# Seven products of half size for the first product of the last stage, in blocks of 640 tokens, with split weight sums kept in DRAM

## The chip, the core and the metric

The kernel runs on one NeuronCore of a Trainium2 chip. The metric is the device time of one execution in microseconds (us). Before the change three runs gave 993.5, 996.51 and 996.72 us; their median is 996.51 us.

The engines: TensorE (PE in the profile; PEld is its weight load), VectorE (DVE), ScalarE (ACT), GpSimd (POOL) and SyncE (SP), which here only issues transfers.

## The reference

Three stages follow one another; each takes the output of the one before.

```python
# 1: attention with a decay, B=4, H=8, S=576, D=64
scores = scale * q @ k.T
out = (scores * gamma ** rel, where rel >= 0) @ v            # -> x (2304, 512)
# 2: mixture of experts, E=8, F=1024, two experts for each token
logits = x @ w_gate;  noise_scale = log1p(exp(x @ w_noise))
top2 of logits + noise_scale * noise;  w = softmax(top2)
out[token] += w * (relu(x @ w1[e]) @ w2[e])                   # -> x (2304, 512)
# 3: the last stage, F2=2048
h = x @ w_in                                                  # (2304, 2048)
return (h * cos(h)) @ w_out                                   # (2304, 512)
```

All is fp32. The kernel keeps the accuracy by splitting: each operand of a large product is written as a high part, rounded to TensorE's fp32r format, and a low part, the rest. A product then takes three matrix products: high x high, low x high, high x low.

## The kernel before, in words

**Order.** Each engine has one program, written out by hand; semaphores order them. An engine does its instructions in the order of its program, so an instruction that waits holds up all behind it. SP issues its transfers in program order too, all on one queue.

**Attention** (to about 130 us) also fills the tables that route the tokens. It scatters the rows of x to slots in DRAM, sorted by expert (`x_slots`).

**Experts** (about 130 to 575 us). The work is cut into units: one expert and 640 slots. A unit goes through the eight 128-wide parts `f` of the hidden width. For each `f` TensorE does `product1` (L1303, 24 matmuls of 320 columns) of the next part and `product2` (L1321, 15 matmuls of 512 columns) of this one, and for `f` under 5 it transposes one tile of 128 rows for the next unit (L1209). ScalarE does `relu`, then `w_high` (L674), which rounds the next expert's weight chunk, 128x1024, and `x_high` (L634). VectorE does the low parts: `h_low` (L1032), `w_low` (L1038) and `x_low` (L1017). SP loads the chunks (`load_ring`, L435) and the rows (`load_rows`, L429), and stores a unit's results to `y_slots` (`store_rows`, L442). The results go out at the end of a unit, and the 256 KB loads `gath` for the unit after next's transposes come behind these stores in SP's order.

**The last stage** (from 576 us). Blocks of 384 tokens (`TPB` = 3 tiles of 128). GpSimd gathers the two result rows of each token (L586); ScalarE and VectorE weigh and add them (`prepare` L731, `combine` L1109). TensorE transposes the sum (L1394), and `prepare_high` (L737) and `combine_low` (L1116) split it. Then for each of the 16 parts `f` of the hidden width `mlp_step` does:

- TensorE: 12 matmuls of 384 columns into one of four PSUM banks (L1458), then 9 of 512 columns (L1477) of the part three steps back (`MLP_LAG`).
- ScalarE and VectorE, for one part of `h`: round `h/2pi` to whole turns (L797, L1165), subtract them (L1168), `Abs` (L802), `Sin` with a bias of pi/2 (L804), the product with h (L1173), and the split of the result (L809, L1176). These steps depend on each other in this order.
- The 16 weight chunks of this stage are loaded and split into `w_hi`, `w_lo`, `w2_hi` and `w2_lo` (`w_high_last` L755, `w_low_last` L1054) during the last unit and the first block. They stay in SBUF for all six blocks.

## Time and profile before

| what | us |
|---|---|
| three runs | 993.5, 996.51, 996.72 |
| profiled execution | 993.64 |
| its span | 991.7 |
| busy TensorE | 973.3 (98%) |
| busy VectorE | 486.5 (49%) |
| busy ScalarE | 425.3 (43%) |
| last stage, first product to the last matmul's end | 575.99 to 987.0 |

1.94 us of the execution lie around the span. "Busy" of TensorE counts from a matmul's start to its modelled end. The matmuls overlap, so the mean duration of one is longer than the distance from one start to the next; what a matmul costs in a row of them is read from the chain of waits, as the length of a piece divided by its count.

### The profile page before, as it was taken

What the parts mean: (1) busy time and instruction counts of PE and PEld (TensorE: products, weight loads), DVE (VectorE), ACT (ScalarE), POOL (GpSimd) and SP (SyncE); (2) the same over time, 40 slices, a digit from 0 to 9 for tenths busy, and PEclk for the clock granted to TensorE, in tenths of its full rate; (3) what the DMA queues carried; (4) which work ended last, traced back from release to release, by engine and by line L of the source; (5) the groups of instructions that cost most, each with busy time, mean ns of one, the idle gap of its engine ahead of it and who ended that gap; (6) DMA issues with size and microseconds to landing.
All of it is one profiled execution on the core that took longest, in us unless ns stands there. A gap on an engine that the chain in (4) does not pass through costs nothing.

```text
span 991.7 us, 17311 instructions
## 1 busy us (share of the span) xinstructions
PE 973.3 (98%) x6108; PEld 879.6 (89%) x6108; DVE 486.5 (49%) x944; ACT 425.3 (43%) x779; POOL 104.1 (10%) x106
## 2 busy tenths in 40 slices
PE   8999899999999999999999989999999999999997
PEld 7989789898989988898989979999999999999996
DVE  4788644333334333433434475555555555555554
ACT  1445334233233332332334465555455554545553
POOL 2276500000000000000000231000000001010000
PEclk9999999999999999999999999999999999999999
DMA  9988444436263542626315641010010101010000
GB/s 363 345 321 302 162 165 154 160 109 212 82 225 114 159 168 97 221 95 196 125 71 175 225 164 43 22 46 30 21 53 21 53 21 42 32 42 21 32 0 33
DMA packets 64359, 122.02 MB, mean 123 GB/s; under 512 B 5696, under 2 KB 31552, under 8 KB 64320
## 3 DMA queue, kind: packets, MB, share of 16 engines
q1 hardware_dynamic: 58080, 101.05, 29.7%
q0 software_dynamic: 6240, 20.45, 6.2%
q8 instruction: 25, 0.41, 0.2%
q14 instruction: 14, 0.11, 0.0%
HBM read 83.73 MB, written 37.75 MB: 122 GB/s over the span
## 4 chain that ended last, share of the span: by engine, by line
PE 86%; DMA 5%; issue 3%; POOL 2%; SPq 2%; DVE 1%; ACT 1%; ACTq 0%; POOLq 0%; DVEq 0%
PE ps L1458 20%; PE ps L1477 20%; PE ps L1303 15%; PE ps L1321 14%; PE ps L1209 2%; DMA gath<-x_slots 2%; PE ps L1339 2%; PE ps L1224 2%; PE ps L1407 2%; PE ps L1351 2%; PE ps L1247 2%; PE ps L1419 2%; DMA y_slots<-y_sb 1%; PE ps L1239 1%; POOL x_slots L540 1%
## 5 line engine op out<-in xcount | busy, mean ns | idle before, releaser
L1303 PE MATMUL ps<-xs,w_hi 128*128 (+1 forms) x784 | 182.9, 312 | 0.0
L1038 DVE TENSOR_TENSOR w_lo<-raw,w_hi 128x1024 fp32r<-128x1024 f32 x48 | 58.8, 1225 | 170.8 <-ACT w_hi L674 170.8
L1303 PEld LDWEIGHTS ps<-xs,w_hi 128*128 128x128 f32 x784 | 133.1, 188 | 0.8
L1458 PE MATMUL ps<-x_hi,w_hi 128*128 (+1 forms) x384 | 130.8, 341 | 0.1
L1458 PE MATMUL ps<-x_hi,w_lo 128*128 (+1 forms) x384 | 129.1, 336 | 0.0
L1458 PE MATMUL ps<-x_lo,w_hi 128*128 (+1 forms) x384 | 129.1, 336 | 0.0
L797 ACT ACTIVATE turns<-ps 128x384 f32<-128x384 f32 x96 | 47.2, 491 | 184.2 <-PE ps L1458 184.2
L1303 PE MATMUL ps<-xs,w_lo 128*128 (+1 forms) x392 | 121.2, 309 | 0.0
L1165 DVE TENSOR_SCALAR turns<-turns 128x384 f32<-128x384 f32 x96 | 37.3, 388 | 168.1 <-ACT turns L797 168.1
L1477 PE MATMUL ps<-w_hi,g_hi 128*128 128x512 f32 x288 | 112.6, 391 | 2.1 <-DVE g_lo L1176 2.1
L1477 PE MATMUL ps<-w_hi,g_lo 128*128 128x512 f32 x288 | 113.3, 393 | 0.0
L1477 PE MATMUL ps<-w_lo,g_hi 128*128 128x512 f32 x288 | 113.3, 393 | 0.0
L674 ACT ACTIVATE w_hi<-raw 128x1024 fp32r<-128x1024 f32 x48 | 50.8, 1059 | 141.3 <-PE ps L1321 107.8
L1321 PE MATMUL ps<-w_hi,hs_lo 128*128 128x512 f32 x245 | 96.2, 393 | 0.0
L1321 PE MATMUL ps<-w_lo,hs_hi 128*128 128x512 f32 x245 | 96.2, 393 | 0.0
L1321 PE MATMUL ps<-w_hi,hs_hi 128*128 128x512 f32 x245 | 95.8, 391 | 0.0
L668 ACT ACTIVATE hs_hi<-ps 128x320 fp32r<-128x320 f32 x98 | 42.3, 437 | 79.3 <-PE ps L1303 79.3
L1458 PEld LDWEIGHTS ps<-x_hi,w_hi 128*128 128x128 f32 x384 | 72.1, 188 | 3.7 <-issue 0.5
L1458 PEld LDWEIGHTS ps<-x_hi,w_lo 128*128 128x128 f32 x384 | 72.1, 188 | 3.1
L1303 PEld LDWEIGHTS ps<-xs,w_lo 128*128 128x128 f32 x392 | 73.7, 188 | 0.8
L1458 PEld LDWEIGHTS ps<-x_lo,w_hi 128*128 128x128 f32 x384 | 72.1, 188 | 0.0
L586 POOL DMA_INDIRECT y<-y_slots,pos_now x42 | 41.8, 995 | 276.3 <-PE ps L1394 266.9
(167 smaller groups left out, 1649.4 us busy)
## 6 DMA issues: line engine op xcount, KB each, us to landing
raw<-weights SPq DMA_DIRECT2D x80, 512.0 KB
y_slots<-zeros_sb SPq DMA_DIRECT2D x42, 256.0 KB, 3.6
gath<-x_slots SPq DMA_DIRECT2D x40, 256.0 KB, 3.5
y_slots<-y_sb SPq DMA_DIRECT2D x40, 256.0 KB, 2.1
qk<-qk SPq DMA_DIRECT2D x18, 512.0 KB
kv<-kv SPq DMA_DIRECT2D x18, 512.0 KB
out<-out_sb SPq DMA_DIRECT2D x18, 256.0 KB, 2.1
x_slots<-zeros_sb SPq DMA_DIRECT2D x8, 256.0 KB, 7.7
```

The source lines that it names most:

```text
L586: nc.gpsimd.indirect_dma_start(out=y[j][:, :], out_offset=None, in_=y_slots, in_offset=bass.IndirectOffsetOnAxis(ap=pos_now[:, k, j:j + 1] ...
L668: nc.scalar.activation(hs_hi[:, par, half * HALF:(half + 1) * HALF], ps[5 + half][:, 0:HALF], ACT.Relu).then_inc(relu_done, 1)
L674: nc.scalar.activation(w_hi[:, f * CHUNK:(f + 1) * CHUNK], raw[:, f % 2, :], ACT.Copy).then_inc(hi_done, 1)
L797: nc.scalar.activation(turns[f % 2][:, :], h_bank(f)[:, 0:TB], ACT.Copy, scale=PER_TURN, bias=ROUND).then_inc(turn_done, 1)
L1038: tt(w_lo[:, at], raw[:, f % 2, :], w_hi[:, at].bitcast(F32), ALU.subtract).then_inc(split_done, 1)
L1165: ts(whole[:, :], whole[:, :], -ROUND, None, ALU.add).then_inc(whole_done, 1)
L1209: last_one = nc.tensor.transpose(x_bank(g, j)[:, k * BLK:(k + 1) * BLK], gath[j][:, k * P:(k + 1) * P], ident)
L1224: last_one = nc.tensor.matmul(ps[half][0:C, n * C:(n + 1) * C], qk_sb[t % 3][rows, 1, n, :], qk_sb[t % 3][rows, 0, n, :], start=True, stop ...
L1303: last_one = nc.tensor.matmul(ps[5 + half][:, 0:HALF], w[:, at:at + P], xs[:, bass.ds(g % 2, 1), a, k, half * HALF:(half + 1) * HALF].rear ...
L1321: last_one = nc.tensor.matmul(ps[j][:, :], a[:, f % 2, j * BLK:(j + 1) * BLK], w[:, at:at + DM], start=f == 0 and i == 0, stop=f == FE - 1 ...
L1458: last_one = nc.tensor.matmul(h_bank(f)[:, 0:TB], w[:, cols], a[:, bass.ds(par, 1), k, :].rearrange("p a s -> p (a s)"), start=k == 0 and ...
L1477: last_one = nc.tensor.matmul(ps[j][:, :], a[f2 % 2][:, rows], w[:, cols], start=f2 == 0 and i == 0, stop=f2 == FT - 1 and i == 2)
```

## The change

**Arithmetic.** The first product of the last stage is written as a product of 2 x 2 blocks: x is cut by tokens and by the 512 features into halves, `w_in` by features and by pairs of 128-wide hidden parts. A scheme of Strassen's kind (with sums that are shared, in Winograd's way) then needs seven products of blocks, where the plain one needs eight, and sums of the operands and of the results. `h` comes out as h1, h2, h3 and h4, the four quarters for two parts and two halves of the tokens.

**Blocks.** `SIZES = (3, 5, 5, 5)`: a first block of 384 tokens, done with plain products, then three of 640 with the scheme, so halves of 320 columns. A *slot* is one pair of hidden parts of one block; there are 8 to a block and 32 in all. `p` is the number of the slot in its block.

**Weights.** The 2 x 2 blocks of each pair, their four sums and all low parts are made during units 1 to 4 of the experts stage (`pair_high`, `pair_low`), from a buffer `raw_pair`, and written to DRAM (`w1_pairs`, `w2_pairs`) by SP (`next_pair`). The last stage reads them again for every slot (`load_w1`, `load_w2`). The splits of the last unit and the first block are gone. The factor 1/2pi is folded into the gates, 2pi into the copy of the results, and the subtraction of whole turns is one instruction of VectorE, where it was two. The gather copies no indices ahead of it. The loops over blocks are written out.

```diff
+SIZES = (3, 5, 5, 5)
...
+A11, A12, A22, S3, S2, S4, S1 = range(0, 7 * Q_W, Q_W)
...
+ORDER = ((A11, 0), (A12, 1), (S2, 4), (S3, 5), (A22, 6), (S1, 3), (S4, 2))
...
+DRAINED = (0, 1, 2, 3, 4, 6, 7)
...
+            def store_pair(i):
+                sp.wait_ge(pair_lo, 3 * (i + 1))
+                sp.dma_start(w1_pairs[i], stage1[i % 2][:, :, :].bitcast(F32)).then_inc(pair_out[i % 2], 16)
+                sp.dma_start(w2_pairs[i], stage2[i % 2][:, :, :].bitcast(F32)).then_inc(pair_out[i % 2], 16)
...
+            def next_pair(i):
+                store_pair(i)
+                if i + 2 < FP:
+                    load_pair(i + 2)
...
                     load_ring(g, f, e_next)
+                    if isinstance(g, int) and 1 < g <= PREP_UNITS + 1 and f == 1:
+                        next_pair(2 * (g - 1) - 1)
+                    if isinstance(g, int) and g <= PREP_UNITS and f == 5:
+                        next_pair(2 * (g - 1))
...
+            def load_w1(slot):
+                if slot >= 2:
+                    sp.wait_ge(p_done, products_before(slot - 1))
+                cols = slice(0, A_W) if slot < FP else slice(Q_W, 2 * A_W)
+                sp.dma_start(w1_of(slot).bitcast(F32), w1_pairs[slot % FP][:, :, cols]).then_inc(w1_in[slot % 2], 16)
```

TensorE's seven products of a slot:

```diff
+            def strassen(slot, o):
+                b, i, n = slot // FP, products_before(slot) + o, HALVES[slot // FP]
+                at, m = ORDER[o]
+                if o == 0:
+                    pe.wait_ge(w1_in[slot % 2], 16 * (slot // 2 + 1))
+                if slot % FP == 0:
+                    pe.wait_ge(x_lo_done, 7 * (b - 1) + o + 1)
+                if slot == FP and o < 2:
+                    pe.wait_ge(g_done, i - 1)
+                elif o == 2:
+                    pe.wait_ge(p1_copied, slot - FP + 1)
+                else:
+                    back = (i - 2 - products_before(FP)) // 7
+                    pe.wait_ge(drained, 7 * back + DRAINED[(o - 2) % 7])
+                w, x = w1_of(slot), x_of(b)
+                for k in range(2):
+                    cols = slice(at + k * P, at + (k + 1) * P)
+                    for j, (hl, a) in enumerate(((0, 0), (1, 0), (0, 1))):
+                        last_one = nc.tensor.matmul(p_bank(i)[:, 0:n], w[:, hl, cols], x[:, a, m, k, :],
+                                                    start=k == 0 and j == 0, stop=k == 1 and j == 2)
+                last_one.then_inc(p_done, 1)
...
+            BEHIND = {10: (1, 1, 2, 1, 2, 2, 1), 6: (1, 1, 1, 1, 1, 1, 0)}
```

VectorE's order in a slot of 640 tokens (`p_done` comes from TensorE, `turn_done` and `sin_done` from ScalarE):

```diff
+                    reduce(slot - 1, 3)
+                    g_low(slot - 1, 2)
+                    product(slot - 1, 3)
+                if slot < SLOTS:
+                    dve.wait_ge(p1_copied, slot - FP + 1)
+                    drain(slot, 1, h_sb[0], p1_sb)
+                if slot > FP:
+                    g_low(slot - 1, 3)
+                if slot == SLOTS:
+                    for j in range(1, SIZES[NBK - 1], 2):
+                        rows_out(NBK - 1, j)
+                    break
+                if p == 1 and b > 1:
+                    rows_out(b - 1, 3)
+                reduce(slot, 0)
+                drain(slot, 2, u2, p1_sb)
+                product(slot, 0)
+                g_low(slot, 0)
+                dve.wait_ge(drained, drained_before(slot) + 2)
+                drain(slot, 3, u3, u2)
+                if p == 0 and b > 1:
+                    rows_out(b - 1, 1)
+                if b + 1 < NBK:
+                    ahead(b, p)
+                dve.wait_ge(drained, drained_before(slot) + 3)
+                drain(slot, 4, h_sb[1], u3, True)
+                reduce(slot, 1)
+                drain(slot, 5, u4, u2)
+                drain(slot, 5, h_sb[2], u3)
+                product(slot, 1)
+                reduce(slot, 2)
+                g_low(slot, 1)
+                dve.wait_ge(drained, drained_before(slot) + 5)
+                drain(slot, 6, h_sb[3], u4)
+                if p == 0 and b == 1:
+                    rows_out(0, 1)
+                product(slot, 2)
```

`ahead(b, p)` makes the split tokens of the next block; VectorE's share of it in block 0 from slot 5 on, and then in blocks 1 and 2:

```diff
+                    if p == 5:
+                        x2_low(1, 0)
+                    if p == 6:
+                        x2_low(1, 1)
+                        for i in range(4):
+                            x2_sum(1, i)
+                    if p == 7:
+                        for at in range(2, 7):
+                            x2_low(1, at)
```

```diff
+                    if p < 5:
+                        combine(first + p)
+                    if p == 4:
+                        x2_low(b + 1, 0)
+                        x2_low(b + 1, 1)
+                    if p == 5:
+                        x2_sum(b + 1, 0)
+                        x2_sum(b + 1, 1)
+                    if p == 6:
+                        x2_sum(b + 1, 2)
+                        x2_sum(b + 1, 3)
+                        x2_low(b + 1, 2)
+                    if p == 7:
+                        for at in range(3, 7):
+                            x2_low(b + 1, at)
```

In block 0 VectorE's order for a slot is `product` and `g_low` of the last slot's second part, `reduce`, `product` and `g_low` of part 0, `ahead`, `reduce` of part 1; ScalarE follows the same order with `turn`, `cosine` (Abs and Sin) and `g_high`. `second` is the old L1477 for one tile and one hidden part: 3 matmuls of 512 columns. `BEHIND` says how many of them follow each of the seven products; there are 10 in a slot of 640 tokens and 6 in one of 384. `drain` is an addition of VectorE that takes a product out of its PSUM bank (two banks, `ps5` and `ps6`, in turn); the first product is copied by ScalarE (`p1_copied`).

The first place is TensorE in the last stage: the end of one step of `mlp_step` before. `x_hi` and `x_lo` are the split tokens, `w_hi` and `w_lo` the weights, `g_hi` and `g_lo` the split h cos(h).

```order
L1458 MATMUL ps<-x_hi,w_hi 128x384
L1458 MATMUL ps<-x_hi,w_lo 128x384
L1458 MATMUL ps<-x_lo,w_hi 128x384
L1466 REGISTER_ALU
L1477 MATMUL ps<-w_hi,g_hi 128x512 [waits g_split]
L1477 MATMUL ps<-w_lo,g_hi 128x512
L1477 MATMUL ps<-w_hi,g_lo 128x512
```

And the same engine within a slot of the block of 640 tokens, with the changed order:

```order
L1831 MATMUL ps<-x_odd,w_sb 128x320 x6
L1749 MATMUL ps<-table_sb,y_2 128x128 x4
L1831 MATMUL ps<-x_odd,w_sb 128x320 x6
L1845 MATMUL ps<-w_sb,g_hi 128x512 x2
L1845 MATMUL ps<-w_sb,g_lo 128x512
L1831 MATMUL ps<-x_odd,w_sb 128x320 x6
```

What stood as 12 and 9 matmuls in a row now stands as 6 and 3, or 6 and twice 3; a transpose (L1749) falls between two products.

The second place is VectorE in the loop over blocks before: one step, with the split of a transposed tile.

```order
L1165 TENSOR_SCALAR turns<-turns 128x384 [waits turn_done]
L1168 SCALAR_TENSOR_TENSOR angle<-ps,turns 128x384 [waits g_split,whole_done]
L1173 TENSOR_TENSOR angle<-ps,angle 128x384 [waits sin_done]
L1176 TENSOR_TENSOR g_lo<-angle,g_hi 128x384 [waits g_hi_done]
L1116 ISA [waits x2_hi_done]
L1116 TENSOR_TENSOR x_lo<-ps,x_hi 128x4x128
```

Its counterpart is the middle of the last slot of block 1, where the split tokens of block 2 (`x_even`) are made:

```order
L1440 TENSOR_TENSOR angle<-h_sb,angle 128x320 [waits sin_done]
L1445 TENSOR_TENSOR g_lo<-angle,g_hi 128x320 [waits g_hi_done]
L1425 TENSOR_TENSOR u<-ps,u 128x320 [waits p_done,drained]
L1380 TENSOR_TENSOR x_even<-xT_sums,x_even 128x640 [waits x_hi_done] x3
L1380 TENSOR_TENSOR x_even<-xT_raw,x_even 128x640 [waits x_hi_done]
L1423 TENSOR_TENSOR h_sb<-u,ps 128x320 [waits p_done,drained]
L1434 SCALAR_TENSOR_TENSOR angle<-turns,h_sb 128x320 [waits g_split,turn_done]
L1425 TENSOR_TENSOR u<-ps,u 128x320 [waits p_done]
```

The drains (L1425, L1423) that set TensorE's banks free now stand in one queue with the four instructions of 640 columns, and behind waits for ScalarE (`sin_done`, `g_hi_done`).

The third place is SP at the start of a unit of the experts stage, with the change:

```order
L522 DMA gath<-x_slots 128x512
L528 ISA [waits split_done]
L528 DMA raw<-weights 128x1024
L569 DMA w_pairs<-stage_1 128x4096 [waits pair_lo]
L570 DMA w_pairs<-stage_1 128x2048
L565 DMA raw_pair<-pairs 128x2048 [waits pair_lo]
L522 ISA [waits tx_done]
L522 DMA gath<-x_slots 128x512
```

Before, the two `gath` stood there with only a `raw` between them; now two stores and a load of a weight pair go ahead of the third `gath`.

## Rows read from the trace of the kernel before

**Rows 1.** The page: busy engines, GB/s in 40 slices of the span, chain by engine.

```profile
PE 973.3 (98%) x6108; PEld 879.6 (89%) x6108; DVE 486.5 (49%) x944; ACT 425.3 (43%) x779; POOL 104.1 (10%) x106
...
GB/s 363 345 321 302 162 165 154 160 109 212 82 225 114 159 168 97 221 95 196 125 71 175 225 164 43 22 46 30 21 53 21 53 21 42 32 42 21 32 0 33
...
PE 86%; DMA 5%; issue 3%; POOL 2%; SPq 2%; DVE 1%; ACT 1%; ACTq 0%; POOLq 0%; DVEq 0%
```

**Rows 2.** Windows: us, busy PE, PEld, DVE, ACT, POOL, granted clock, DMA share, GB/s.

```profile
0.00:100.00 100.00, 96.64 (x1361) 87.38 (x1361) 73.37 (x194) 42.58 (x71) 45.90 (x44) 1.00 0.91 331
565.00:575.00 10.00, 8.92 (x56) 7.52 (x55) 5.68 (x9) 4.55 (x10) 1.85 (x2) 1.00 0.59 201
776.00:848.00 72.00, 72.00 (x370) 65.39 (x369) 37.92 (x75) 37.19 (x76) 5.88 (x7) 1.00 0.11 33
```

**Rows 3.** Chain of waits, experts stage: start, length, what.

```profile
232.60 2.74 DMA gath<-x_slots
...
250.48 0.44 PE ps L1209 x4
250.91 3.52 PE ps L1303 x24
254.44 3.44 PE ps L1321 x15
```

**Rows 4.** Chain of waits, start of the last stage and its steady part.

```profile
552.75 1.41 PE ps L1419 x6
...
575.99 4.43 PE ps L1458 x24
...
586.05 2.33 PE ps L1477 x9
...
603.37 2.07 PE ps L1477 x9
605.44 2.09 PE ps L1458 x12
...
613.78 0.44 PE ps L1394 x4
```

**Rows 5.** Groups by form, experts stage: count, busy us, mean ns, idle before.

```profile
L1038 DVE TENSOR_TENSOR w_lo<-raw,w_hi 128x1024 fp32r<-128x1024 f32 x41 | 50.2, 1225 | 144.1 <-ACT w_hi L674 144.1
L1032 DVE SCALAR_TENSOR_TENSOR hs_lo<-ps,hs_hi 128x320 fp32r<-128x320 f32 x81 | 38.5, 485 | 36.2 <-ACT hs_hi L668 36.2
L1017 DVE TENSOR_TENSOR xs<-ps,xs 128x512 f32 x25 | 17.0, 682 | 0.0
...
L668 ACT ACTIVATE hs_hi<-ps 128x320 fp32r<-128x320 f32 x80 | 34.6, 437 | 64.4 <-PE ps L1303 64.4
```

**Rows 6.** Groups by form, last stage.

```profile
L804 ACT ACTIVATE angle<-angle,table_sb 128x384 f32<-128x384 f32 x96 | 59.2, 617 | 3.1
L1173 DVE TENSOR_TENSOR angle<-ps,angle 128x384 f32<-128x384 f32 x96 | 53.4, 557 | 7.8 <-ACT angle L804 0.5
L802 ACT ACTIVATE angle<-angle 128x384 f32<-128x384 f32 x96 | 49.6, 516 | 0.0
L1109 DVE SCALAR_TENSOR_TENSOR y<-y,gate 128x512 f32<-128x512 f32 x21 | 15.8, 751 | 4.2 <-ACT y L731 2.4
```

**Rows 7.** Timeline of VectorE, last stage, instructions that wait for nothing.

```profile
592.56 0.55 DVE L1173 TENSOR_TENSOR angle<-ps,angle 128x384 f32<-128x384 f32 x1
593.02 0.55 DVE L1176 TENSOR_TENSOR g_lo<-angle,g_hi 128x384 fp32r<-128x384 f32 x1
```

**Rows 8.** Chain of waits at the end: hand-overs ScalarE to VectorE to TensorE.

```profile
979.46 0.02 issue
979.48 0.47 DVE angle L1173
...
980.52 0.04 issue
```

**Rows 9.** Timeline of the end: the copies of the results.

```profile
987.03 1.08 ACT L793 ACTIVATE out_sb<-ps 128x512 f32<-128x512 f32 x2 [3.50 <-PE ps L1477]
```

792 lines of the change are left out of this document (521 added, 271 removed).

## The prediction, made before the changed kernel ran

> **What bounds the kernel now.** I read the page first. TensorE is busy 98% and is 86% of the chain that ended last; VectorE is half idle [rows 1]. By windows the last stage has TensorE busy for all of 72 us, VectorE for 37.9, ScalarE for 37.2, at 33 GB/s and at a granted clock of 1.00, the 2.4 GHz level [rows 2]. So TensorE's work sets the time there, and work taken from it counts as long as the others keep up. What a matmul costs in a row I take from the chain: 24 of 320 columns in 3.52 us (0.147 each), 15 of 512 in 3.44 (0.230) [rows 3], 12 of 384 in 2.09 (0.174), 9 of 512 in 2.07 (0.230) [rows 4].
>
> **Products, -19.4 us.** For 640 tokens and a pair of hidden parts the plain first product costs 24 x 0.174 x 640/384 = 6.97 us. The new one has 7 x 6 = 42 matmuls of 320 columns, 6.16 us. That is 0.81 less in each of 24 slots, 19.4 in all: an eighth less work, of which the narrower matmuls give back a bit. The second product (30 x 0.230 = 6.90 a slot), the first block and the 18 transposes stay. A slot of 640 tokens is then 13.06 us of TensorE, 13.5 with a transpose (0.44) [rows 4].
>
> **More seams.** Groups are now of 6 and 3 matmuls. A group of 9 costs 2.07 and one of 15 costs 3.44, the same 0.230 each, so a seam costs nothing there; one of 6 took 1.41, up to 0.03 over 6 x 0.230 [rows 3, 4]. With some 10 seams more a slot the bounds are 0 and 24 x 10 x 0.03 = 7 us. I take 0, by the larger groups.
>
> **Do VectorE and ScalarE keep up?** This decides the case. The trace shows no drain, so I price it by VectorE's 0.485 at 320 columns. A copy on ScalarE is 0.437 at 320; Abs and Sin fall from 0.516 and 0.617 at 384 to about 0.46 and 0.56, by the slope of copies [rows 5, 6]. A hand-over between engines takes 0.02 to 0.04 [rows 8]; I take 0.04. Independent instructions of VectorE start 0.46 apart while one lasts 0.55 [rows 7], so at 320 I take 0.42.
>
> In a slot VectorE has 7 drains, 4 `reduce`, 4 `product`, 4 `g_low`: 19 x 0.42 = 8.0 us of 13.06. But its order makes one long chain with ScalarE. From `product` 3 of one slot: drain 1, turn, reduce, Abs, Sin, product 0, g_high, g_low, drains 3 and 4, turn, reduce, Abs, Sin, product 1, g_high, g_low, drain 6, turn, reduce, Abs, Sin, and `product` 3 again. The durations sum to 10.9, 20 hand-overs to 0.8: 11.7 us, 1.3 under TensorE's 13.06. So bare slots (all of block 3) run at TensorE's pace.
>
> The work for the next block stands in that chain, ahead of drain 4. An instruction of 640 columns lies between 0.682 (512) and 1.225 (1024) [rows 5]; by the slope 0.82, or 0.76 from start to start. The chain grows to:
>
> - p=0 to 3: 12.4 to 13.6 against 13.5; about even.
> - p=4: a combine (0.751 [rows 6]) and two lows behind ScalarE: 14.1 against 13.5, 0.6 over.
> - p=5: two sums, 13.2 against 13.1, 0.1 over.
> - p=6: two sums and a low, 14.0, 0.9 over.
> - p=7: four lows, 14.7, 1.7 over.
>
> That is 3.3 over. TensorE takes a bank two products after it was filled; the tightest of these waits, for `p1_copied`, has 0.9 us in hand. So TensorE stands about 2.5 us before each of blocks 2 and 3: **+5 us**. In block 0 a slot is 8.35 us (24 x 0.174 + 18 x 0.230) and the chain 6.7, with 1.9 over in p=6 (a low and four sums, 4.0 us) and 1.6 in p=7 (five lows, 3.9). And the last `reduce` of the block stands behind those five lows. The second product of slot 8 waits for its `product` (g_done): by my times that comes 4.3 us late. **+4.3 us**. The bounds of these 9.3 us: 0, if waits that I add up overlap; 30, if hand-overs cost more (a rival below).
>
> **Start of the last stage, -1.9 us.** Before, TensorE stood 1.1 us of the 10 before the stage [rows 2], waiting for gathered rows. The gather starts about 0.9 us sooner without its index copy, and no weight chunks share the DMA engines with it: -1.1. Then four products of 2.09 would end at 584.35, but the first second product starts at 586.05 [rows 4]: 1.7 lost while weights are split on ScalarE and VectorE. Now none are split there, but with two banks the third product must wait for the whole chain of the first, about 0.9. -0.8. Bounds of both: -2.8 and 0.
>
> **End, -0.5 us.** Two copies took 1.08 us after the last matmul [rows 9]; now the other tiles end sooner and one copy is left, about 0.6. The chain of the last quarter needs 4.1 us and has 5.5 of second products ahead.
>
> **Weight pairs in the experts stage, +2 us.** ScalarE gets 3 instructions of 1024 columns a pair (about 1.06 us each), VectorE 3 (1.225) and 4 small sums, over four `f` of about 7 us. Both are busy under half of the time, and `h_low`, which frees TensorE's bank, has some 3 us in hand; this is hidden. SP is the risk. In units 2 to 5 two stores and a load (2.1 + 1.05 + 1.05 MB) go between the second and the third `gath`. From the first `gath` at 232.60 to the end of the third: 4.2 + 3 x 0.26 + 2 x 0.52 = 6.0 MB. The highest rate on the page is 363 GB/s [rows 1], so 16.6 us, and about 1.7 of latency (a 256 KB `gath` took 2.74 [rows 3]): 18.3. TensorE wants the third `gath` at 250.48, 17.9 later [rows 3]. So it is late by 0.4 four times, or by 3.8 at the 302 GB/s of a busy slice. Bounds 0 and 15; I take +2, near the higher rate. The same traffic at `f`=5 has nothing urgent behind it.
>
> In the last stage a slot loads 1.8 + 1.05 MB in 13.06 us, with gathers and results about 255 GB/s; the first stage moved 331 at a share of 0.91 [rows 2], and each load is issued a slot ahead. Cost 0; without that cover it would be some 5 us a slot, which nothing here suggests.
>
> **Sum.** -19.4 - 1.9 - 0.5 + 5.0 + 4.3 + 2.0 = -10.5 us. Against the profiled 993.6 that gives 983.1. The profiled execution lies at the lower end of the three runs and 2.9 under their median. I do not know at which level the new runs fall, so I add half of that: **984.5 us**.
>
> **Rivals.**
>
> 1. *The chain becomes the bound (slower).* If a hand-over costs 0.10 in place of 0.04, which is open for instructions with two waits, the chain is 12.9 to 13.0 bare and about 14.9 on average with the next block's work. In blocks 1 and 2 that is 16 x 1.6 = 26 us where I count 5: 1005 us. It decides from 0.06 us more per hand-over, or from 0.06 more for each instruction. For it: 20 steps in series and only 1.3 us in hand. Against it: the measured 0.02 to 0.04 [rows 8]. Chance 0.18. A page speaks for it: the Trainium skill, "VectorE: DVE Perf Modes", The DRAIN you can't avoid, has the next instruction wait after each one for its duration less 266 ns. By that rule 19 instructions are 19 x (0.485 + 0.22) = 13.4 us a slot, and VectorE itself would be the bound. The trace disagrees: starts 0.46 apart at a duration of 0.55 [rows 7]. I give it nothing beyond the rival's chance.
> 2. *No stalls at the boundaries, and the third `gath` in time.* All of the 11.3 us that I add are gone: 984.5 - 11 = 973.5. For it: TensorE's waits have slack that a lag uses up before it counts, and VectorE has 5 us idle a slot. Against it: the order is fixed, and slot 7 leaves no slack for slot 8. Chance 0.16.
> 3. *The stores delay the experts stage.* With writes moving slower than the loads by which I set the rate, four units lose 3 us each and the results' stores come late too: +8 to +13, 995 us. For it: no stretch of the trace writes 3 MB in one go. Chance 0.12.
> 4. *The seams cost their upper bound*, 0.03 each: +7, 991.5. For it: the group of six; against it: 9 and 15 alike. It also stands for a small cost of the many waits before groups of three. Chance 0.04.
>
> The forecast has 0.47; 0.03 is for what I don't see. A measurement of this kernel tells a difference of about 0.3% (3 us) from none. Faster by more than that: the forecast, rivals 2 and 4, a little of rival 3: 0.69. Within: 0.12, most of rival 3 and part of what I don't see. Slower: rival 1 and a little: 0.19. The range takes in rival 2 and nearly all of rival 1: 973 to 1004; the forecast's own is 978 to 991.
>
> **What the profile after would show.** Pieces of the chain of 6 matmuls of 320 columns of about 0.88 us, TensorE's slots in blocks 1 to 3 of 13.1 to 13.5 us, block 3 without a gap. Idle time of TensorE with VectorE's drains as releaser (or ScalarE's copy, `p1_copied`) just before blocks 2 and 3, some 2.5 us each, and one of 4 at slot 8 with a `product` as releaser. In the experts stage waits of L1209's successor for `gath` in four units. I am wrong if slots of block 3 take over 13.5 us (then rival 1 holds), if the matmuls of 320 columns take over 0.16, or if the experts stage grows by more than 5 us.

## The result, and the profile after

Seven runs of the changed kernel have a median of 989.95 us (987.93 to 993.93), against 996.03 us for seven of the kernel before. The ratio is 0.9947, with a 95% interval of 0.9926 to 0.9967: faster by about half a per cent, 6 us, where 12 were forecast. The profiled execution took 989.95 us, its span 988.1. The page of the changed kernel, beside [rows 1]; the line of a group gives count, busy us, mean ns, and the idle time before it with what ended it:

```profile
PE 958.0 (97%) x6144; PEld 860.2 (87%) x6144; DVE 562.6 (57%) x1118; ACT 477.4 (48%) x889; POOL 95.0 (10%) x93
...
PE 68%; ACT 8%; DVE 8%; DMA 8%; issue 4%; SPq 2%; POOL 2%; POOLq 0%; DVEq 0%; ACTq 0%
...
L1831 PE MATMUL ps<-x_odd,w_sb 128*128 128x320 f32 x672 | 118.9, 313 | 6.3 <-DVE angle L1440 4.6
```

TensorE has 15 us less to do, but its share of the chain falls from 86% to 68%: ScalarE, VectorE and transfers now hold it up in places. The spans, 991.7 and 988.1 us, split like this. The measured column adds up to their difference within 0.1 us:

| part | forecast | measured |
|---|---|---|
| products of the last stage | -19.4 | -19.2 |
| boundaries to blocks 2 and 3 | +5.0 | +5.6 |
| boundary to block 1 (slots 8 and 9) | +4.3 | +8.4 |
| other stalls of the last stage | -0.8 | -2.8 |
| end | -0.5 | -1.4 |
| start of the last stage, gather | -1.1 | -1.5 |
| weight pairs in units 2 to 5 | +2.0 | +4.5 |
| loop over units written out on SP | 0 | -3.6 |
| pair loads ahead of the first stores | 0 | +6.5 |
| sum | -10.5 | -3.5 |

"Slot" is one hidden pair in one block; slots 0 to 7 are block 0, 8 to 15 block 1. The measured rows come from the starts of slots and units in both traces; the rows of the loop and of units 2 to 5 are told apart by e5_split below.

**The steady part.** The chain of the changed kernel in block 3, from one slot's second group of products to the next slot's (start, length, what):

```profile
912.66 0.88 PE ps L1831 x6
913.54 0.69 PE ps L1845 x3
...
925.74 0.88 PE ps L1831 x6
```

Six matmuls of 320 columns take 0.88 us and three of 512 0.69, as forecast, and a slot is 925.74 - 912.66 = 13.08 us (forecast 13.06). Nothing but TensorE stands in the chain between. VectorE's timeline in block 2 answers to [rows 7], and the groups by form, in 850 to 985 us, to [rows 5, 6]:

```profile
862.79 0.48 DVE L1434 SCALAR_TENSOR_TENSOR angle<-turns,h_sb 128x320 f32<-128x320 f32 x1
863.20 0.48 DVE L1425 TENSOR_TENSOR u<-ps,p_sb 128x320 f32<-128x320 f32 x1
```

```profile
L954 ACT ACTIVATE angle<-angle,table_sb 128x320 f32<-128x320 f32 x40 | 22.5, 563 | 1.3
...
L1440 DVE TENSOR_TENSOR angle<-h_sb,angle 128x320 f32<-128x320 f32 x40 | 19.6, 490 | 14.8 <-ACT angle L954 14.6
```

Starts are 0.41 apart at a duration of 0.48 (taken: 0.42), Sin is 0.563 (0.56), a VectorE step 0.490 (0.485). By the rule of the Trainium skill, "VectorE: DVE Perf Modes", The DRAIN you can't avoid, the second would have started about 0.7 after the first (an estimate by its formula). The same section adds that an instruction that is not held starts earlier, and the trace agrees with this exception, as it did before the change. So the section was no argument for rival 1.

**The first unit of the experts stage.** This is the chain of the changed kernel, where the forecast had no term:

```profile
167.58 6.40 DMA y_slots<-y_sb
...
174.42 0.70 DVE y_sb L1277
...
178.52 2.62 DMA gath<-x_slots
...
181.27 1.11 PE ps L1565 x4
182.38 5.13 PE ps L1659 x24
187.52 3.43 PE ps L1677 x15
190.94 0.44 PE ps L1565 x4
```

The transfers issued in 162 to 182 us (KB each, and the median us from issue to landing), and the windows around the wait (columns as in [rows 2]):

```profile
raw_pair<-pairs SPq DMA_DIRECT2D x2, 1024.0 KB, 8.5
y_slots<-y_sb SPq DMA_DIRECT2D x5, 256.0 KB, 6.4
```

```profile
174.00:180.00 6.00, 1.82 (x7) 1.05 (x6) 2.81 (x4) 2.20 (x4) 0.00 (x0) 0.92 0.33 112
180.00:186.00 6.00, 4.73 (x19) 4.74 (x20) 2.26 (x3) 2.87 (x4) 0.00 (x0) 0.51 0.84 293
```

The same chain of the kernel before:

```profile
168.04 2.10 DMA y_slots<-y_sb
...
173.95 2.69 DMA gath<-x_slots
...
176.77 0.65 PE ps L1209 x4
177.42 3.53 PE ps L1303 x24
```

The first result store takes 6.40 us in place of 2.10, with two pair loads of 1 MB ahead of it on the queue (e1_early tests this). VectorE needs the store's buffer for its next copy of results, SP issues the later stores and then `gath`, and TensorE waits for `gath`: 4.5 us later than before. Behind the wait the granted clock is 0.51, TensorE's 1.2 GHz level. Four transposes take 1.11 us for 0.65 and 24 matmuls 5.13 for 3.53: another 2.0. The Trainium skill, "DMA: Bandwidth & Descriptors", Queues, rings and completion order, says that a DMA engine takes the descriptors of one ring in order. The trace agrees with it: the small store, issued behind the large loads, takes 6.40 us for 2.10.

**Slots 8 and 9.** Chain of the changed kernel:

```profile
648.74 1.99 DVE x_odd L1380 x3
...
650.86 1.56 DVE x_odd L1380 x2
...
654.12 0.57 DVE angle L1440
...
654.82 1.94 PE ps L1831 x6
656.76 1.28 PE ps L1845 x3
...
667.81 0.59 ACT out_sb L968
...
668.53 0.92 PE ps L1845 x3
```

Five low parts (L1380) and the last reduce stand ahead of the product (L1440) that slot 8 waits for: 4.6 us, near the forecast 4.3. Behind this wait, too, TensorE runs at its lower level for a while: the granted clock is 0.50 in 654.8 to 658.8, and six matmuls take 1.94 us for 0.88. The rest of this row, 3.8 us, is taken apart below. At the boundary to block 2 TensorE's timeline has three waits, 0.61 us at 752.15 and these two (idle time in brackets):

```profile
764.36 1.12 PE L1831 MATMUL ps<-x_even,w_sb 128*128 128x320 f32 x6 [0.44 <-DVE h_sb L1425]
766.81 1.12 PE L1831 MATMUL ps<-x_even,w_sb 128*128 128x320 f32 x6 [0.64 <-ACT p_sb L934]
```

**The end.** One copy of 0.60 us follows the last matmul, for 1.08 in [rows 9]:

```profile
984.88 0.60 ACT out_sb L968
```

### The profile page after: what moved, and what is told of

Same layout as the page of the kernel before. It is cut to its first block, busy times and chain, and to the rows that moved or that the text cites. A ratio compares the mean times of both kernels' runs of the same rounds, so it can differ in the third digit from the quotient of the medians.

```text
span 988.1 us, 17016 instructions
## 1 busy us (share of the span) xinstructions
PE 958.0 (97%) x6144; PEld 860.2 (87%) x6144; DVE 562.6 (57%) x1118; ACT 477.4 (48%) x889; POOL 95.0 (10%) x93
## 4 chain that ended last, share of the span: by engine, by line
PE 68%; ACT 8%; DVE 8%; DMA 8%; issue 4%; SPq 2%; POOL 2%; POOLq 0%; DVEq 0%; ACTq 0%
PE ps L1845 13%; PE ps L1659 13%; PE ps L1677 12%; PE ps L1831 10%; DMA gath<-x_slots 5%; PE ps L1762 3%; PE ps L1774 2%; ACT angle L954 2%; PE ps L1809 2%; ACT angle L952 2%; PE ps L1695 2%; DVE angle L1440 2%; PE ps L1580 2%; PE ps L1707 2%; PE ps L1603 2%
## 5 line engine op out<-in xcount | busy, mean ns | idle before, releaser
L1845 PE MATMUL ps<-w_sb,g_hi 128*128 128x512 f32 x576 | 181.2, 396 | 0.9 <-ACT out_sb L968 0.9
L1831 PE MATMUL ps<-x_odd,w_sb 128*128 128x320 f32 x672 | 118.9, 313 | 6.3 <-DVE angle L1440 4.6
L1831 PEld LDWEIGHTS ps<-x_odd,w_sb 128*128 128x128 f32 x672 | 107.8, 190 | 17.7 <-issue 7.0
L1845 PE MATMUL ps<-w_sb,g_lo 128*128 128x512 f32 x288 | 112.7, 391 | 0.0
L1845 PEld LDWEIGHTS ps<-w_sb,g_hi 128*128 128x128 f32 x576 | 101.5, 189 | 10.7 <-issue 1.2
L952 ACT ACTIVATE angle<-angle 128x320 f32<-128x320 f32 (+1 forms) x112 | 53.7, 480 | 41.6 <-DVE angle L1434 40.2
L1445 DVE TENSOR_TENSOR g_lo<-angle,g_hi 128x320 fp32r<-128x320 f32 (+1 forms) x112 | 56.1, 501 | 29.6 <-ACT g_hi L960 22.9
L960 ACT ACTIVATE g_hi<-angle 128x320 fp32r<-128x320 f32 (+1 forms) x112 | 53.7, 480 | 36.2 <-DVE angle L1440 34.1
L1440 DVE TENSOR_TENSOR angle<-h_sb,angle 128x320 f32<-128x320 f32 x96 | 47.2, 491 | 36.4 <-ACT angle L954 35.2
L954 ACT ACTIVATE angle<-angle,table_sb 128x320 f32<-128x320 f32 (+1 forms) x112 | 63.9, 571 | 3.6
```

The source lines that it names most:

```text
L952: nc.scalar.activation(a, a, ACT.Abs).then_inc(abs_done, 1)
L954: nc.scalar.activation(a, a, ACT.Sin, scale=-2.0 * np.pi, bias=tab("half_pi")).then_inc(sin_done, 1)
L960: nc.scalar.activation(g_part(g_hi, slot, q), angle[c % 4][:, 0:width(slot)], ACT.Copy).then_inc(g_hi_done, 1)
L1440: tt(angle[c % 4][:, 0:n], h_of(slot, q)[:, 0:n], angle[c % 4][:, 0:n], ALU.mult).then_inc(g_done, 1)
L1445: tt(g_part(g_lo, slot, q), angle[c % 4][:, 0:n], g_part(g_hi, slot, q).bitcast(F32), ALU.subtract).then_inc(g_split, 1)
L1831: last_one = nc.tensor.matmul(p_bank(i)[:, 0:n], w[:, hl, cols], x[:, a, m, k, :], start=k == 0 and j == 0, stop=k == 1 and j == 2)
```

## The experiments

A time without an interval is that of one profiled run. "After" is the changed kernel. Single runs differ by more than some of the effects below. The last transpose ahead of the experts stage's first unit comes at 153.8 to 156.9 us in the seventeen traces, with no order by the edits: 154.05 in the trace of after, but 156.26 in e1_early, 156.07 in e10_eos and 156.92 in e11_best. So the readings go by the lengths of slots and units, and not by the whole time.

### The experts stage

**e1_early**: the first two pair loads go out between weight chunks, well before the results are stored.

```diff
             for f in range(2, FE):
                 load_chunk(RING + f, FE + f)
+                if f in (5, 6):
+                    load_pair(f - 5)
...
-            for i in range(2):
-                load_pair(i)
             for j in range(TPU):
                 store_rows(0, j)
```

> The two first loads of weight pairs (1 MB each) are issued between the chunk loads of the first unit, before its last two chunks, and no longer just ahead of the stores of the first unit's results. My theory: these two loads hold up the first store (6.4 us to land, 2.1 before the change), with it the copies of results 3 and 4, the gath behind them and TensorE, which then runs at the lower clock for a while; so the first transpose after the first unit comes at about 176.8 as before the change (181.3 with it), the one after it at 184.4 (190.9), and the execution is 6 to 6.5 us shorter than the changed kernel: 983.5. Rival (the work of pairs on ScalarE and VectorE, or their traffic in units 1 to 5, holds TensorE up): under 1.5 us.

984.98 us, the median of four runs (983.42 to 985.59), ratio to before 0.9904 (0.9888 to 0.9921). The first store lands after 2.09 us again. The windows:

```profile
174.00:180.00 6.00, 4.51 (x24) 3.56 (x23) 2.12 (x3) 0.80 (x3) 0.00 (x0) 1.00 0.66 230
180.00:186.00 6.00, 6.00 (x37) 5.51 (x36) 3.75 (x5) 3.25 (x5) 0.00 (x0) 1.00 0.74 273
```

From the last transpose of the unit ahead to the second one of the first unit it takes 30.4 us, as before (30.3; after 36.7). The added wait and the low clock are both gone: 6.3 us, as the theory said; the rival falls. The whole time falls by 5.0 us only, and the first 156 us of its trace are 2.2 us longer than those of after.

**e5_split**: the next pair is loaded at `f`=1, the last one stored at `f`=3.

```diff
-                    if isinstance(g, int) and 1 < g <= PREP_UNITS + 1 and f == 1:
-                        next_pair(2 * (g - 1) - 1)
+                    if isinstance(g, int) and 1 < g <= PREP_UNITS and f == 1:
+                        load_pair(2 * (g - 1) + 1)
+                    if isinstance(g, int) and 1 < g <= PREP_UNITS + 1 and f == 3:
+                        store_pair(2 * (g - 1) - 1)
```

> In units 2 to 5 the 1 MB load of the next pair stays after the second gath, and the 3 MB of stores come after the fourth. My theory: the third gath then has 1 MB ahead of it instead of 4 MB and lands in about 6 us in place of 15.1, so the transposes that waited for it (about 0.6 us in four units by the distance from unit to unit: shifts of +6.54, +7.13, +8.32, +8.65 against before) don't: 1.5 to 2 us shorter in the experts stage. Rival (the fifth gath is now late, since the stores stand ahead of it): the same 2 us, one transpose later.

985.9 us. Five units (fifth transpose to fifth transpose) take 289.1 us; after, 293.6. In the changed kernel the third `gath` of unit 2 is issued at 242.34 and lands 15.14 us later, 19.1 us after the issue of the unit's first at 238.40 (forecast 18.3):

```profile
242.34 15.14 DMA gath<-x_slots
```

With the edit it lands after 7.34 us, and no transpose waits for it. The theory holds and the rival (a late fifth `gath`) falls; the size is larger: 4.5 us, where the prediction said 2 and this expectation 1.5 to 2.

**e12_flat**: the kernel before with SP's loop over units 1 to 5 written out.

```diff
-            with sp.Fori(1, E - 2) as g:
+            for g in range(1, E - 2):
                 unit_loads(g)
```

> The kernel before with one edit: the loop over units 1 to 5 in the list of SyncE is written out, as the changed kernel has it; it issues the same transfers. In the changed kernel a unit without weight pairs takes 57.8 us, in the kernel before 58.6. My theory: the loop's own turn-round on SyncE stands between the last store of one unit and the first gath of the next, and TensorE waits for it; so five units take 0.7 to 0.8 less each here, 3.5 to 4 in all, ratio 0.996. Rival: the difference comes from what the changed kernel moved elsewhere (the index copies, the weight splits), and this kernel takes the same time as before.

991.2 us, ratio 0.9958 (0.9943 to 0.9974): 4.0 us by the medians. Five units take 289.7 us for 292.7, so 3.0 by the units. The rival falls. So a part of the changed kernel's gain has nothing to do with its products.

### The boundary to block 1

**e2_order**: VectorE's and ScalarE's work on the next tokens is spread; low parts 5 and 6 stand behind the product.

```diff
                 if slot == FP:
                     product(slot - 1, 1)
                     g_low(slot - 1, 1)
+                    x2_low(1, 5)
+                    x2_low(1, 6)
```

> Only the order in the last slot of block 0 differs from the changed kernel: ScalarE does two of the four roundings of 640 columns after Abs and Sin of the last quarter, VectorE one low part after the last reduce and two after its product and g_low. My theory: the wait of the second product of slot 8 (4.6 us for g_done) is the chain behind the low parts of that slot, so it falls by 2 to 3 us, and the low clock after it (granted 0.62 in the 6 us from 652, costing about 2 us) goes too: slot 8 takes 13 to 15 us where it took 18.0. Rival (the wait comes from the DMA or from the lag of earlier slots): slot 8 stays above 17.

988.65 us; slots 8 and 9 take 14.64 + 15.42 = 30.06 us (after 32.63). The wait for the product is down from 4.6 to 2.4, at a granted clock of 1.00:

```profile
653.93 1.12 PE L1838 MATMUL ps<-x_odd,w_sb 128*128 128x320 f32 x6 [2.39 <-DVE angle L1443]
```

The distance from drain 1 of slot 8 to that of slot 9, the length of VectorE's and ScalarE's chain in slot 8, is 12.70 us here, and VectorE waits for no product of TensorE in it:

```profile
656.84 0.48 DVE L1428 TENSOR_TENSOR h_sb<-ps,p_sb 128x320 f32<-128x320 f32 x1
...
669.54 0.48 DVE L1428 TENSOR_TENSOR h_sb<-ps,p_sb 128x320 f32<-128x320 f32 x1
```

**e3_banks**: slot 8's first two products go to banks 3 and 4, so that they don't wait for `g_done`.

```diff
-            return ps[5 + i % 2]
+            return ps[{2 * FP: 3, 2 * FP + 1: 4}.get(i, 5 + i % 2)]
```

> The first two products of slot 8 go to PSUM banks 3 and 4, free at that time, instead of 5 and 6; the third and fourth then wait for the products of block 0 that the first two waited for. My theory: two banks are what makes the chain of block 0's last quarter late; with 3.1 us more before it is needed the wait falls from 4.6 to 1.5 us and the clock stays up: slot 8 about 13 us in place of 18.0. Rival (the low parts themselves are late, x_lo_done): the wait only moves, slot 8 stays at 17 to 18.

989.6 us; slots 8 and 9 take 14.84 + 15.44 = 30.28 us. Two quite different edits end at 30: free banks move the wait to the next drains (`u` 1.7, `angle` 1.4 us) and to slot 9. The chain in slot 8 is 12.69 us here as well. So something that neither edit touches sets the time from 30 down.

**e13_out**: e11_best (below) with ScalarE's copy of the first result tile ahead of Abs and Sin.

```diff
                 g_high(slot, 1)
+                if p == 0 and b == 1:
+                    rows_out(0, 0)
                 cosine(slot, 2)
-                if p == 0 and b == 1:
-                    rows_out(0, 0)
```

> e11_best with one instruction moved: ScalarE copies the first result tile of block 0 out of its bank before Abs and Sin of the third quarter of slot 8, not behind them. In e9_spread and e11_best slot 9 takes 15.4 us where its neighbours take 13.5, and TensorE's second product waits there for this copy (out_sb). Theory: the copy's place is the whole of it; the wait of 1.9 us shrinks by the Abs and Sin of 1.04 us that stand ahead of it, and slots 8 and 9 take 29.0 together in place of 30.0: 973.4 - 1.0 = 972.4. Rival: the copy waits for the last second products of slot 7, and those come late because slot 8 stood; then the place changes nothing and slots 8 and 9 stay at 30.0.

973.08 us, the median of five runs (972.67 to 974.49), ratio 0.9773 (0.9759 to 0.9786), against 973.4 for e11_best: the same. Slots 8 and 9 take 29.04 us for 29.99, which looks like the theory. But e9_spread (below), which has the copy at its old place, takes 29.06. What differs is the granted clock, 0.72 in one and 1.00 in the other. The wait ahead of slot 8's second product is 1.91 us in e9_spread and 1.93 in e11_best, with the same code in this stage, and the 6 us behind it, first in e11_best and then in e9_spread, read (columns as in [rows 2]):

```profile
644.00:650.00 6.00, 6.00 (x26) 5.49 (x27) 3.83 (x8) 3.38 (x8) 0.00 (x0) 0.72 0.60 244
```

```profile
651.00:657.00 6.00, 6.00 (x35) 5.54 (x36) 4.60 (x9) 4.29 (x9) 0.00 (x0) 1.00 0.61 247
```

So the moved copy gains nothing that shows, and the match with 29.0 is luck. Nor does the rival hold as written, since slots 8 and 9 didn't stay at 30.0. The wait for `out_sb` is gone from slot 9, but its 15.41 us are not: a wait for `p_sb` stands in its place. What stays is the chain; VectorE's timeline of e13_out has drain 1 of slots 8 and 9:

```profile
644.52 0.49 DVE L1433 TENSOR_TENSOR h_sb<-ps,p_sb 128x320 f32<-128x320 f32 x1 [0.18 <-ACT p_sb L937]
...
658.18 0.48 DVE L1433 TENSOR_TENSOR h_sb<-ps,p_sb 128x320 f32<-128x320 f32 x1
```

In slot 8 the chain takes 13.66 us here, two low parts included that e9's order put into it. In the changed kernel the distance is 13.95:

```profile
656.87 0.49 DVE L1425 TENSOR_TENSOR h_sb<-ps,p_sb 128x320 f32<-128x320 f32 x1 [1.04 <-PE ps L1831]
...
659.68 0.49 DVE L1425 TENSOR_TENSOR u<-ps,p_sb 128x320 f32<-128x320 f32 x1 [1.29 <-PE ps L1831]
...
670.82 0.48 DVE L1425 TENSOR_TENSOR h_sb<-ps,p_sb 128x320 f32<-128x320 f32 x1
```

TensorE's own work in slot 8 is 42 x 0.147 + 18 x 0.230 + 0.44 = 10.74 us, since the second products beside it are still those of block 0. So the chain sets the length of this slot. But the 13.95 us are not all chain: VectorE waits in them for TensorE's slow products, 1.29 us ahead of drain 2 and 0.41 ahead of drain 4. Without the low clock the same instructions take 12.7 (e2_order, e3_banks and e10_eos). The 3.8 us behind the wait thus split into 12.7 - 10.74 = 2.0 for the chain and 1.8 for the low clock, 1.25 of these within the chain and the rest about drain 1. The first is read in three runs; the second is what is left. In the six traces in which slot 8's code is that of after, it takes 17.05 to 18.29 us, at granted clocks of 0.80 to 0.90.

### A long wait by itself

**e14_stall** and **e15_long**: e11_best with additions on spare tiles, each waiting for the last, ahead of drain 4 in two slots of block 3 (5 and 9 of them; then 12 and 17).

```diff
+                for _ in range({26: 5, 29: 9}.get(slot, 0)):
+                    link(tt(y2[0][:, :], y2[2][:, :], y2[2][:, :], ALU.add))
                 dve.wait_ge(drained, drained_before(slot) + 3)
```

> e11_best with additions on spare tiles before drain 4, each waiting for the last, 5 in slot 26 and 9 in slot 29 (block 3, where a slot takes 13.07 and nothing else disturbs it). They are 128x512 and should take about 0.7 us each: 3.5 and 6.3 us. 1.5 us of that is in hand, so TensorE should stand about 2.0 and 4.8 us. This measures the cost of a long wait by itself. Theory A (the clock is granted lower for some us after a wait of over 4 us, as at slot 8 of the changed kernel, and that adds about 2 us to the wait): slot 26 grows by 2.0 at a granted clock of 1.00; slot 29 and 30 grow by 4.8 + 2 together at a granted clock of about 0.6 behind the wait. Theory B (the lower clock in the changed kernel came with slot 8's DMA traffic and low parts, not with the wait): both grow by their wait alone, 2.0 and 4.8, at 1.00.

> e14_stall with longer waits: 12 additions before drain 4 in slot 26 and 17 in slot 30, at 0.73 us each 8.8 and 12.4 us. In e14_stall 6.6 us of additions cost 4.8 us, in pieces of 2.6, 0.4 and 0.6 and an uneven rest, and the granted clock stayed at 1.00. Here the largest single wait is about 4.8 us in slot 26 and 8.5 us in slot 30. Theory A (a single wait of over 4 us is followed by a lower granted clock, and by matmuls at half their pace): slots 26 and 27 grow by 8.8 - 1.8 = 7.0 for the wait and by 1 to 3 more at a clock of about 0.5 to 0.8; slots 30 and 31 by 12.4 - 1.8 = 10.6 and again 2 to 3 more. Theory B (no wait lowers it, something else at slot 8 and at the first unit did): 7.0 and 10.6 alone, at 1.00.

e14_stall, 979.04 us: slots 26 and 27 grow by 1.8 us together, 29 and 30 by 4.8. The waits come in pieces, the largest 2.64, and the clock stays at 1.00 in block 3. With no single wait of the length that theory A asks for, this run decides nothing:

```profile
937.31 1.14 PE L1854 MATMUL ps<-x_odd,w_sb 128*128 128x320 f32 x6 [2.64 <-DVE h_sb L1431]
...
941.40 1.14 PE L1854 MATMUL ps<-x_odd,w_sb 128*128 128x320 f32 x6 [0.36 <-DVE h_sb L1433]
...
943.85 1.16 PE L1854 MATMUL ps<-x_odd,w_sb 128*128 128x320 f32 x6 [0.61 <-ACT p_sb L937]
```

e15_long, 990.74 us: TensorE's timeline at slot 26, and the windows there:

```profile
899.11 1.97 PE L1854 MATMUL ps<-x_odd,w_sb 128*128 128x320 f32 x6 [4.82 <-DVE h_sb L1431]
```

```profile
894.00:898.00 4.00, 0.29 (x2) 0.00 (x0) 3.80 (x7) 0.00 (x0) 0.00 (x0) 0.83 0.00 0
898.00:902.00 4.00, 2.89 (x9) 2.70 (x10) 3.10 (x7) 2.12 (x5) 0.00 (x0) 0.50 0.00 0
```

Around a single wait of 4.82 us the clock falls to its lower level, with no transfer in either window: theory A on the clock. But slots 26 and 27 grow by 19.53 + 13.67 - 2 x 13.07 = 7.06 us, the bare wait of 7.0 that theory B gave, and slots 30 and 31 by 10.5 (10.6). The matmuls behind the wait lose about 2.2 us. My reading is that at the higher clock TensorE would have waited for the chain instead: the waits of 0.36 and 0.61 us that follow in e14_stall are missing behind this one. No run holds the clock and leaves the wait.

The length of a wait alone doesn't decide. Ahead of slot 8 the clock fell in e11_best, e14_stall and e15_long, behind waits of 1.93, 1.92 and 1.91 us, and not in e9_spread and e13_out, behind 1.91 and 1.93. In e7_all it fell about a wait of 2.37, in e2_order not, at 2.39. At this place the fall isn't free: in the five traces with e9's order slots 8 and 9 take 29.9 to 30.3 us with it and 29.0 to 29.1 without. What decides whether it falls, no run shows.

The Trainium skill, "TensorE: Matmul & The Clock Gate", HAM oscillation — how this bites in real kernels, counts half of the time at the low clock as lost. The trace agrees roughly at the first unit, where nothing but TensorE's own work stands behind the wait (2.0 us), and not in block 3.

### The boundaries to blocks 2 and 3

**e4_pool**: the four sums (L1375) of blocks 2 and 3 go to GpSimd.

```diff
+            def pool_sums(b):
...
+                for i in range(4):
...
+                    nc.gpsimd.tensor_tensor(t[:, i, :, :], first, second, ALU.subtract).then_inc(x_sums, 1)
```

> GpSimd makes the four sums of 640 columns for blocks 2 and 3 (1.31 us each for 512 columns before the change, so some 1.65); VectorE has them no longer and its low parts spread over the last two slots of a block. My theory: VectorE's queue is what stretches these slots: in the changed kernel slots 5, 6 and 7 of block 1 and slot 0 of block 2 take 13.24, 13.24, 13.94 and 14.99, in place of 13.07 and 13.51; that is 2.7 us over a boundary. It falls to under 0.7, for two boundaries 4 us. Rival (ScalarE's share of the chain, or a GpSimd that slows VectorE through the shared port): no change, or slots that grow by the port.

991.47 us, no gain. Slots 14 and 15 and the next one take 14.91 + 13.11 + 14.24 = 42.26 us; after, 13.24 + 13.94 + 14.99 = 42.17. The timelines of GpSimd and of VectorE:

```profile
730.59 1.58 POOL L735 TENSOR_TENSOR xT_sums<-xT_raw 128x640 f32<-128x640 f32 x1 [4.87 <-ACT xT_raw L894]
...
735.67 1.70 POOL L735 TENSOR_TENSOR xT_sums<-xT_sums,xT_raw 128x640 f32<-128x640 f32 x1
```

```profile
732.41 1.75 DVE L1450 SCALAR_TENSOR_TENSOR angle<-turns,h_sb 128x320 f32<-128x320 f32 x1 [0.54 <-ACT turns L961]
734.08 0.48 DVE L1441 TENSOR_TENSOR u<-ps,u 128x320 f32<-128x320 f32 x1
...
735.86 1.86 DVE L1450 SCALAR_TENSOR_TENSOR angle<-turns,h_sb 128x320 f32<-128x320 f32 x1
```

The sums take 1.6 to 1.8 us each, for VectorE's 0.82, and end at 737.4. While they run, `reduce` (L1450) takes 1.75 and 1.86 us on VectorE where it takes 0.48 in the same trace without them, and both times it ends 0.35 us behind the end of a sum. A drain (L1441), which reads one of its inputs from PSUM, keeps its 0.48. TensorE's waits in slot 14 are 0.52 us at 738.58 and 0.80 at 741.22, and the first instruction that needs the sums starts later, at 744.8. So slot 14 grows by 1.7 us because GpSimd's work slows VectorE's, as the rival had it, and what VectorE saves in the next two slots (1.6 us) goes there. The same shows at the next boundary (1.40 and 1.86 us) and in e7_all.

**e9_spread**: the same work, in other places. One item a slot stands behind drain 2, where VectorE waits for Abs and Sin anyway; low parts that are needed late are made in the new block's first slot.

```diff
                 drain(slot, 2, u2, p1_sb)
+                if 0 < b < NBK - 1 and p == 6:
+                    x2_sum(b + 1, 2)
+                if 0 < b < NBK - 1 and p == 7:
+                    x2_low(b + 1, 3)
+                if b > 1 and p == 0:
+                    x2_low(b, 6)
+                if slot == FP:
+                    x2_low(1, 5)
                 product(slot, 0)
                 g_low(slot, 0)
+                if slot == FP:
+                    x2_low(1, 6)
```

> The changed kernel with the sums and low parts of the next block's tokens in other places of VectorE's order (and the high parts to match on ScalarE), same work. For blocks 2 and 3 one item of each slot stands behind drain 2, where VectorE waits for Abs and Sin anyway; two low parts instead of four stand ahead of drain 4 in the last slot, and the last low part is made in the first slot of the new block. For block 1 two sums move from slot 6 to slot 7, and low parts 3 to 6 stand where VectorE waits for ScalarE, the last two inside slot 8. My theory (the stalls at a boundary are the chain of VectorE and ScalarE made longer by the items that stand in it): the chain of slots 5 to 7 comes under TensorE's 13.1, so slot 7 and the next slot 0 take about 13.1 and 13.5 us (13.94 and 14.99 in the changed kernel), 2 us less for each of two boundaries, and slots 8 and 9 take about 27.5 together (32.63), 5 less: 990 - 9 = 981. Rival (VectorE's idle time is spent on waiting that another item cannot use, so an item costs the same wherever it stands, as the sums on GpSimd suggested): boundaries as they were, 990 to 986.

980.58 us, for an expected 981. Slot 15 and the next take 13.11 + 13.52 us for 13.94 + 14.99, slots 8 and 9 13.62 + 15.44 for 17.96 + 14.67; this sum of 29.1 is 1.6 over the expected 27.5. In all of blocks 1 to 3 only slots 8 and 9 are now over TensorE's own time by more than 0.3 us. At the boundaries to blocks 2 and 3 the theory holds and the rival falls: what counts is whether an item stands in the chain or in VectorE's idle time.

### The margin of the chain

**p1_pad** and **p3_pad**: one and three additions of 128x512 ahead of drain 4, in seven slots of block 3.

```diff
+                if b == NBK - 1 and p > 0:
+                    for spare in (y2[0], y2[1], y1[0])[0:3]:
+                        tt(spare[:, :], y2[2][:, :], y2[2][:, :], ALU.add)
```

> In slots 1 to 7 of block 3 VectorE gets one spare addition of 512 columns (about 0.69 us, 0.62 from start to start) ahead of drain 4; its result is not used. Slots of block 3 take 13.07 us in the changed kernel. My reading of the chain (11.7 us, so 1.3 in hand): they stay at 13.07. Rival 1 (the chain is at or near the bound): they grow by about 0.5 each.

> As p1_pad with three spare additions, 1.8 to 1.9 us a slot; their results are not used. With 1.3 us in hand slots grow by about 0.5 each once the slack of 0.9 is used up, to some 13.6; with no hand they grow by 1.8 each, to 14.9; with 2 or more in hand they stay at 13.07.

With one (989.46 us) slots stay at 13.07. With three (994.72 us; 1.86 us of VectorE from start to start) they are 13.45: 0.37 more, so 1.5 us were in hand and the chain is 11.6 us. The prediction had 11.7 and 1.3.

### Together

**e7_all** (e1, e2, e3 and e4), **e10_eos** (e1, e5 and e2) and **e11_best** (e1, e5 and e9), with no other edit.

> e1_early, e2_order, e3_banks and e4_pool together. If the four places add up as read (6.3 + 5 with the clock + 4 of the boundaries, of which slot 8's two edits overlap) it is 14 to 15 us shorter than the changed kernel: 975. If GpSimd's sums don't help: 979. If the loads of pairs are not the cause in the experts stage: 981 or more.

> The changed kernel with the edits of e1_early, e5_split and e2_order together. Their gains, measured one by one, are 6.3, 4.5 and 2.6 us. If they add: 989.95 - 13.4 = 976.5. The rival is that they don't, because the two edits of the weight pairs shift the same transfers: the second would give less once the first is made, and the sum would be 978 to 981. The trace tells by the time from the first unit's transposes to each later unit's.

> The changed kernel with three edits together: the first two loads of weight pairs ahead of the experts stage's stores (as e1_early), stores and loads of weight pairs in separate places (as e5_split), and the order of e9_spread in the last stage. If the terms add: 989.95 - 6.3 - 4.5 - 9 = 970. If moving the items gives nothing at the boundaries to blocks 2 and 3, 976 to 979.

e7_all: 980.81 us (980.44 to 982.42), ratio 0.9855 (0.9837 to 0.9873). Its slots 8 and 9 take 30.03 us, no less than with e2 or e3 alone. But the clock fell here ahead of slot 8 and in those two it didn't, so whether the two add isn't shown. The boundaries to blocks 2 and 3 take what they do with e4 alone, no less than in after.

e10_eos: 978.49 us, 2.0 over the expected 976.5. The part ahead of the first unit ran 2.0 us longer than in the trace of after (156.07 for 154.05), one of the differences between single runs named above. Beside that the three gains add.

e11_best: 973.4 us (971.02 to 974.39), ratio 0.9775 (0.9762 to 0.9789). With e13_out it is the fastest here, 2.2% under the kernel before and 16 us under the changed one. Its slots 8 and 9 take 30.0 us, 2.5 more than I expected, and that is the largest part of the 3.4 us over 970; in e13_out, without the low clock there, it is 29.0.

## Why the prediction was half right

**Direction and main term: right.** The whole gain is half of the forecast one. The products give 19.2 of 19.4 us, the seams cost nothing (rival 4 is out), and drains, turns and cosine keep up: chain 11.6 us for a forecast of 11.7 (p3_pad). That refutes rival 1. The section of the Trainium skill that I named for it has an exception that I left out, as said above. The stalls ahead of blocks 2 and 3 are 5.6 us for 5.0, and e9_spread shows their cause to be the forecast one: items that stand in the chain.

**The step that failed: SP's order.** The prediction said of the weight pairs "SP is the risk" and then counted the bursts in units 2 to 5 only. The diff also puts the first two pair loads ahead of the first unit's stores, and this has the shortest way to TensorE: store, result copy, stores, `gath`, transposes. It costs 6.5 us, 4.5 of wait and 2.0 of low clock (e1_early takes 6.3 of them back), more than any other missing term. The prediction's own sign of being wrong was met: from the last transpose ahead of the first unit to the first product of the last stage it takes 5.7 us more than before, where 5 was the limit. Rival 3 named stores that delay the experts stage, but by slow writes in four units, not by loads ahead of stores in the first.

**Mis-sized: the third `gath`.** I added up 6.0 MB over the page's highest rate, which gave 0.4 us a unit, and took +2. Measured, in unit 2 it landed 19.1 us after the issue of the first `gath` and not 18.3; the transposes that need it came 1.6, 1.5 and 1.1 us late in units 2 to 4 and in time in unit 5, and the term is 4.5 us (e5_split). My own other rate, that of a busy slice, would have given 15.

**Mis-sized: slots 8 and 9.** The wait of 4.6 us is near the forecast one of 4.3, but not by the working as it stands: the delays of 1.9 and 1.6 us in p=6 and 7 don't follow from its own numbers (6.7 + 4.0 and 6.7 + 3.9 against 8.35 give 2.35 and 2.25), and 24 x 0.174 + 18 x 0.230 is 8.32. The other 3.8 us are two things that I left out. TensorE's work in slot 8 is 10.74 us, while the chain there, with a combine and a result copy in it, takes 12.7: 2.0 us. I had compared chain and products only in slots of 13.06 to 13.5. The low clock behind the wait is the other, about 1.8 us by difference; no run changes the clock alone, but slots 8 and 9 of e11_best and e9_spread, with one code and two clocks, differ by 0.9 us.

**Missed gain: the written-out loop.** 3.6 us in the changed kernel, 3.0 to 4.0 in the kernel before (e12_flat). The prediction followed no instruction between a unit's last store and its first `gath`, though the edit stood in the diff. This gain hides as much of the other misses.

**Not settled.** The 2.0 us that I have too little at "other stalls of the last stage" aren't placed by any run. The traces show a part: TensorE's wait near the stage's start is 0.98 us for 1.48, and one of 0.61 us at 980.56, near the end of the kernel before, has no counterpart. Over TensorE's own time, slots 8 and 9 are still 5.7 us in e11_best and 4.8 in e13_out.

The profile of before was an execution at the lower end of its runs, 993.64 us. So the traces differ by 3.7 us and the medians by 6; the table explains the former.

## What to carry to other kernels

Where a diff adds transfers to a queue, list every instruction it is put ahead of, the first use in a prologue included, and follow the nearest one to the engine that sets the time. Compare a chain of helpers with TensorE's work slot by slot, not with the steady slot: it decides where the slot is shortest. Before you give a helper's work to a third engine, look whether that engine's instructions stretch the helper's (e4_pool). Work for the next block belongs where the helper waits for its partner; in the chain it costs its full length, in the gap nearly nothing.

## What the runs showed of the hardware

- Around single waits of 4.6 to 8.5 us of TensorE its granted clock fell to 0.50. Around waits of 1.9 to 2.4 us it fell in four traces and not in four others, with the same code in some of them. Whether the low clock costs time depends on what TensorE would otherwise have waited for: 2.0 us at the first unit, 0.9 in slots 8 and 9 behind a wait of 1.9, none in block 3.
- A loop on SyncE costs 0.6 us (by the units) to 0.8 us (by the medians) a round in e12_flat, where TensorE waits for the first transfer of the next round.
- GpSimd takes 1.56 to 1.83 us for a difference of 128x640 in fp32, VectorE 0.82. While GpSimd does them, VectorE's `reduce` of 128x320 with both inputs in SBUF takes up to 1.86 us in place of 0.48; a drain with one input in PSUM takes its usual 0.48 (e4_pool).
